# FFT convolution with a mixture-of-experts layer: half of the t stores issued by SP, and the constants loaded by SP

## What is computed

```python
def _attn_ref(x, filt_r, filt_i):          # x: 8 batches x 3072 x 256, float32
    X = np.fft.rfft(x, axis=1)
    Y = X * (filt_r + 1j * filt_i)[None]
    return np.fft.irfft(Y, n=x.shape[1], axis=1)

def _moe_ref(x, w_gate, w1, w2, capacity): # 8 experts, 256 -> 1024 -> 256, capacity 768
    logits = x @ w_gate
    expert_idx = np.argmax(logits, axis=1) # gate_w: softmax weight of that expert
    # each expert takes its first `capacity` rows in order; all other rows stay zero
    h = np.maximum(np.einsum('ecd,edf->ecf', disp, w1), 0.0)
    y = np.einsum('ecf,efd->ecd', h, w2)
    # out[i] = gate_w[i] * y[expert, slot] for rows that were kept
```

## Time and profile before

| | |
|---|---|
| three runs | 547.15, 548.21, 555.39 us |
| profiled execution | 550.09 us |
| its span, first to last instruction | 548.3 us |
| mean granted TensorE clock | 0.963 of full |
| busy: TensorE, its weight loads | 472.4 (86%), 376.8 us (69%) |
| busy: VectorE, ScalarE, GpSimd | 222.1 (41%), 205.8 (38%), 216.8 us (40%) |
| moved by DMA | 119.72 MB, mean 218 GB/s |

### The profile page before, as it was taken

One profiled execution on the slowest core, in us unless ns is written; L12 is line 12 of the kernel. 1 busy time (PEld: TensorE's weight loads), 2 busy tenths in 40 slices (PEclk: granted clock), 3 DMA queues, 4 the chain that ended last, 5 costly groups with the idle time before them and its releaser, 6 DMA issues.

```text
span 548.3 us, 9488 instructions
## 1 busy us (share of the span) xinstructions
PE 472.4 (86%) x3806; PEld 376.8 (69%) x3806; DVE 222.1 (41%) x335; ACT 205.8 (38%) x362; POOL 216.8 (40%) x190
## 2 busy tenths in 40 slices
PE   5446666999988986989888998999999999999994
PEld 1123223245544553459888998999999999998994
DVE  7025103233344579757925522253413434232210
ACT  2301322345533633445215444253633535243221
POOL 7080100000000000274545778755678565775212
PEclk9959979899998999999999999999999999999998
DMA  8989978889759646799931316943069331491001
GB/s 285 334 311 408 409 255 264 286 291 298 254 185 340 217 153 210 237 391 405 364 111 40 123 41 238 390 135 133 30 233 394 132 116 49 158 362 58 30 22 43
DMA packets 64532, 119.72 MB, mean 218 GB/s; under 512 B 7760, under 2 KB 35296, under 8 KB 64480
## 3 DMA queue, kind: packets, MB, share of 16 engines
q1 hardware_dynamic: 33168, 70.95, 36.8%
q0 software_dynamic: 9824, 25.33, 12.8%
q10 hardware_dynamic: 21488, 22.75, 12.2%
HBM read 60.78 MB, written 58.23 MB: 217 GB/s over the span
## 4 chain that ended last, share of the span: by engine, by line
PE 62%; DMA 13%; DVE 8%; issue 6%; ACT 5%; ACTq 3%; SPq 2%; POOL 0%; POOLq 0%; DVEq 0%
PE back L1288 21%; PE wide L1274 10%; PE bank L1274 10%; PE back L484 6%; PE low L517 4%; DMA t_scratch<-t_out 4%; DMA u_scratch<-v_out 3%; PE low L499 3%; PE wide L471 3%; ACTq L681 2%; DVE pq L796 2%; PE low L652 2%; PE bank L532 2%; ACT t_out L674 2%; DMA w_raw<-in_w 1%
## 5 line engine op out<-in xcount | busy, mean ns | idle before, releaser
L1288 PE MATMUL back<-w2h,hh 128*128 128x256 f32 x384 | 109.7, 286 | 0.0
L1288 PE MATMUL back<-w2l,hh 128*128 128x256 f32 x384 | 108.6, 283 | 0.0
L1288 PE MATMUL back<-w2h,hl 128*128 128x256 f32 x384 | 108.6, 283 | 0.0
L796 DVE TENSOR_TENSOR pq<-wide,fab 128x1024 f32<-128x1024 f32 x45 | 55.0, 1223 | 123.8 <-PE wide L471 119.1
L1099 DVE SCALAR_TENSOR_TENSOR hl<-wide,hh 128x384 fp32r<-128x384 f32 x64 | 34.7, 555 | 119.6 <-ACT hh L1051 83.6
L1188 POOL DMA_INDIRECT out<-o_out,token x48 | 50.5, 1052 | 81.5 <-ACT o_out L1060 60.4
L1288 PEld LDWEIGHTS back<-w2l,hh 128*128 128x128 f32 x384 | 73.6, 192 | 0.1
L1288 PEld LDWEIGHTS back<-w2h,hl 128*128 128x128 f32 x384 | 73.6, 192 | 0.0
L1288 PEld LDWEIGHTS back<-w2h,hh 128*128 128x128 f32 x384 | 73.6, 192 | 0.0
L1160 POOL DMA_INDIRECT g_in<-y_rows,token x48 | 52.6, 1095 | 33.1 <-DVE token L967 17.4
L1060 ACT ACTIVATE o_out<-back,o_gate 128x256 f32<-128x256 f32 x48 | 22.9, 476 | 102.1 <-PE back L1288 97.4
(11 more groups left out here) (131 smaller groups left out, 778.8 us busy)
## 6 DMA issues: line engine op xcount, KB each, us to landing
out<-zero SPq DMA_DIRECT2D x24, 1024.0 KB
w_raw<-in_w SPq DMA_DIRECT2D x14, 1024.0 KB
u_scratch<-v_out ACTq DMA_DIRECT2D x48, 192.0 KB, 4.0
t_scratch<-t_out ACTq DMA_DIRECT2D x30, 256.0 KB, 6.9
z_in<-t_scratch SPq DMA_DIRECT2D x24, 256.0 KB, 3.9
x_in<-in_x POOLq DMA_DIRECT2D x12, 512.0 KB, 15.1
x_in<-in_x SPq DMA_DIRECT2D x6, 512.0 KB, 6.2
z_in<-t_scratch SPq DMA_DIRECT2D x24, 128.0 KB, 4.9
```

What stands on the lines that cost most here:

```text
L796: nc.vector.tensor_tensor(pq[:, n % 3], spectrum(t, h)[:, :, 0, :].unsqueeze(2).to_broadcast([P, 2, 2, D]), fab[:, h], ALU.mult).then_inc( ...
L1288: mm = nc.tensor.matmul(ps[4 + (b * ST + s) % 2][:, 0:D], hx[:, b % 2, f, s * P:(s + 1) * P], wt[:, k, f, :], start=(f == 0 and m == 0), s ...
```

## The change

The second of the two t stores of every chunk (a = 1, the odd partitions) is issued by SP and no longer by ScalarE, and the five loads of constants as well. SP waits for the same count of t_evac as ScalarE does. Batch 0's six stores stand on SP behind table group 0; those of batch 1 lie around z_load(0, 7), those of batch 2 in steps g = 0 to 2 of stage 1, with the v loads behind the third. The constants are issued after the last store of batch 1 and ahead of z_load(1, 0).

```diff
+        def t_store(eng, t, c, a):
+            at = a * 32 + c * 2 * CH if c < 4 else A1 + a * 16 + (c - 4) * 2 * CH
+            buf = v_in if t == 0 and c >= 3 else t_out
+            eng.wait_ge(t_evac, t * 12 + 2 * c + 2)
+            dst = zt[t, at:at + 2 * CH].rearrange("(n r) (p d) -> (r p) n d", r=2, d=D)
+            eng.dma_start(dst, buf[a:P:2, c % 3]).then_inc(t_written[c % 3], 16)
+
+        def t_stores(sp, t, first, last):
+            for c in range(first, last):
+                t_store(sp, t, c, 1)
...
+        def load_constants(sp):
+            sp.wait_ge(set_up, SET_UP)
+            sp.nop(nofuse=True)
+            sp.dma_start(wai[:, :], wai_d).then_inc(consts, 16)
+            sp.dma_start(sq[:, :, :], sq_d).then_inc(consts, 16)
+            sp.dma_start(wgs[:, :, 0:E], wg.rearrange("(h p) e -> p h e", p=P)).then_inc(consts, 16)
+            sp.dma_start(rows[:, :, :], row_d).then_inc(consts, 16)
+            sp.dma_start(nums[:, :], num_d).then_inc(consts, 16)
+
         def sp_stage(sp, t, ai):
+            late = A_FROM[t] > 0
             for g in range(NG):
                 n = g + ZB
+                if not late:
+                    if g == 0:
+                        t_stores(sp, t + 1, 0, 1)
+                    elif g == 1:
+                        t_stores(sp, t + 1, 3, 4)
+                    elif g == 2:
+                        t_stores(sp, t + 1, 4, NCH)
+                elif n == NG - 1:
+                    t_stores(sp, t + 1, 0, 2)
+                elif n == NG:
+                    t_stores(sp, t + 1, 2, NCH)
+                if t == 0 and n == NG:
+                    load_constants(sp)
                 if n < NG:
                     z_load(sp, t, n)
                 else:
                     z_load(sp, t + 1, n - NG)
+                if not late and g == 0:
+                    t_stores(sp, t + 1, 1, 3)
                 if ai is not None:
...
             if h == 1:
-                act.wait_ge(t_evac, t * 12 + i + 1)
-                for a in range(2):
-                    at = a * 32 + c * 2 * CH if c < 4 else A1 + a * 16 + (c - 4) * 2 * CH
-                    dst = zt[t, at:at + 2 * CH].rearrange("(n r) (p d) -> (r p) n d", r=2, d=D)
-                    act.dma_start(dst, buf[a:P:2, c % 3]).then_inc(t_written[c % 3], 16)
+                t_store(act, t, c, 0)
...
                 load_tables(sp, 0)
+                t_stores(sp, first, 0, NCH)
                 sp.wait_ge(gaps_set, r + 1)
...
-                def stage(t, a, ai, rt):
-                    act_stage(act, t, a, ai, rt)
-                    if t == 0:
-                        act.dma_start(sq[:, :, :], sq_d).then_inc(consts, 16)
-                        act.dma_start(wai[:, :], wai_d).then_inc(consts, 16)
-                        act.dma_start(wgs[:, :, 0:E], wg.rearrange("(h p) e -> p h e", p=P)).then_inc(consts, 16)
-                        act.dma_start(rows[:, :, :], row_d).then_inc(consts, 16)
-                        act.dma_start(nums[:, :], num_d).then_inc(consts, 16)
-                stages(first, last, stage)
+                stages(first, last, lambda t, a, ai, rt: act_stage(act, t, a, ai, rt))
```

## The result

Over twenty runs of each kernel, the changed one has a median of 546.58 us and the kernel before 550.85 us. The ratio is 0.9918, with a 95% interval of 0.9892 to 0.9944: a gain of 4.5 us, where 6.6 were forecast. The ratios leave out executions more than 1.5% above the shortest of the same kernel, the medians count all. Three more sets of runs, on three chips, gave 0.9973 [0.9934, 1.0011], 0.9959 [0.9923, 0.9995] and 0.9921 [0.9884, 0.9959]. The mean of the four is 0.9943, some 3.1 us. Two sets of the kernel before against itself gave 1.0032 and 0.9973, so a single set doesn't tell 0.3% from nothing. The changed kernel is faster, by a little under half of what was forecast.

What follows compares the result with a forecast made beforehand. Transfers and their issue were taken to set the pace before 117 us, TensorE's own work behind it. 0.9 + 4.0 + 1.7 = 6.6 us off the median of 548.21 gave 541.6 us, range 535 to 547.5.

Steps and rivals of the forecast that it cites:

- Batch 0: 0 to 27 us: fewer store issues on ScalarE bring the last landing earlier; 0.9 us, ends 0 and 2.9.
- the slack of 1.1 us: End of batch 0: the DMA work left at 24 us could be done by 25.8, 1.1 us ahead of the landing.
- Stage 0: Batch 1, 57 to 91 us: halves in two queues release chunk 3's copy 5.0 us earlier; gain 4.0 us, ends 1.0 and 6.9.
- SP's issue of the constants: After batch 1's last store: ends by 82 us, five microseconds ahead of the landing, and costs nothing; without that cover, 4.1 us.
- Stage 1: Batch 2, 95 to 117 us: one store issue less per chunk removes most of TensorE's waits; 1.7 us, ends 0 and 3.5.
- rival B: Both clock dips, in stage 0 and at the start of stage 1, shrink too: 12.6 us gained, 535.6 us; chance 0.16.
- the move of the constants: Start of stage 1: taking the constants off ScalarE looks like 4 us and is nothing, as TensorE works without a gap.
- the sum: Whole kernel: 0.9 + 4.0 + 1.7 = 6.6 us gained, all before 117 us.
- Behind 117 us: From 117 us to the end: the path is TensorE's own work, so the earlier gain comes out nearly whole.
- A: Stage 0: landings stay, since all transfers share 16 DMA engines; only shorter issues gain, 1.0 us there; 544.6 us; chance 0.25.
- C: Stage 1: a longer wait keeps the clock at 1.2 GHz through batch 2; 4.9 us slower, 553 us; chance 0.06.
- The bound of 2%: Whole kernel: a difference under 2% (11 us) is about what can't be told from no change; chance of that 0.82.

Runs made afterwards that it cites:

- consts_back: The changed kernel with the five loads of constants back on ScalarE at the end of stage 0; 0.9898 of the kernel before, median 555.54 us.
- busy_last: The changed kernel with three unused TensorE products of 512 columns added in the last stage; 0.9896 of the kernel before, median 542.73 us.
- all_on_sp: The changed kernel with both t stores of every chunk issued by SP, none by ScalarE; 0.9963 and 0.9871 of the kernel before in two sets.

## Why the prediction went as it did

**Batch 0, forecast 0.9 us, measured 0.1.** The first z load is at 27.25, 27.26, 26.97 and 26.98 us, before at 27.12, 27.23 and 27.19. ScalarE's part came nearly as worked out (last issue at 20.66 instead of 22.97, 2.3 us where 2.9 were worked out), the engines were full, and the last stores took 6.4 us instead of 4.0. What failed in this term is the slack of 1.1 us that I saw between the work left at 24 us and the landing: with the stores issued earlier, the share from 24 to 27 us is still 0.58 (0.61 before), and the landing stays. That one slow engine among the 16 is waited for would explain it, but is not shown.

**Stage 0, forecast 4.0 us.** The rows fit the mechanism, the halves in two queues and ScalarE's ending last; but batch 0 alone, with both halves in one queue, has part of the gain, so it isn't shown to be the whole cause. The sizes were off. SP's half took 8.3 us, not 6, and ScalarE's 10.0 and more, not 8.4. Chunk 3's release is at 68.03, 69.79, 68.73 and 68.84 us, 3.3 us earlier in the mean than 72.44, 72.65 and 71.44, where 5.0 were forecast. The z load is 3.6 us earlier in the mean (6.0 in the first profile, 1.9 to 3.6 in the others, against the mean of before, 91.4), where 4.9 were forecast, batch 0 included. SP's issue of the constants, forecast to end by 82 us, ended at 87.4 and 88.3 in the third and second profiles, 1.2 to 1.3 us ahead of the z load: it still cost nothing, but with no 5 us to spare.

**Stage 1, forecast 1.7 us, measured 3.5.** From z load to wai the four profiles take 21.02, 22.14, 21.97 and 24.08 us, mean 22.3; before 25.8. My sum kept the dip at 96 to 100 us. It was absent in three of four, so rival B's term was real here; and with it gone, the move of the constants, costed at nothing, began to count, as `consts_back` has it. The part alone (25.33 us) is worth nothing, as forecast: the error was to cost it for the schedule before and not for the one that the rest of the change makes.

**Up to 117 us** this adds up to 7.1 us in the mean and 5.8 without the first profile, close to the 6.6 of the sum, by terms that err in both directions: the sum was near by luck. `busy_last` is the same kernel up to there and has both old dips (0.50 in 72 to 76 and in 96 to 100 us) and 114.50 us; with it the mean is 6.2 us.

**Behind 117 us, forecast 0.** Here the prediction failed: "what is won before 117 us should therefore come out of the end nearly whole". In the last three profiles 2.3 us are gone by the first w_raw load, in last stages of 114.2 to 116.8 us instead of 113.6. What is left there, 3.5 us, agrees with the 3.1 us of the timed sets; with the lucky first profile it would be 5.6. The step that failed is the reading of the path: TensorE's being busy for 30 of 30 us in stage 1 said nothing of the last stage, where it waits for v and for VectorE. The chain of the kernel before shows that wait, in two transfers that the earlier trace rows stops short of:

```profile
157.82 2.89 DMA u_scratch<-v_out
161.32 4.92 DMA x_in<-u_scratch
```

Behind it the granted clock fell to 0.74 from 164 to 168 us already then. So the term of the last stage was put at nothing without a look at it; it came out at 1.4 us against the change in the mean of four profiles. Why the clock falls deeper or twice in some executions of the changed kernel stays open.

**The rivals.** A had the size nearest to the median, for a wrong reason: its landings were to stay, and chunk 0's pair released the copy at 68.0 to 69.8 us instead of 71.4 to 72.6. B's two dips are gone in three of four profiles, but a low window stands at 76 to 84 us in their place (0.57 in the first, 0.50 in the second and third), and only the first execution (540.95 us) comes near B's side. C wasn't seen in stage 1. The bound of 2% for what can be told was also too coarse: four sets of runs tell 0.6% from nothing, and a faster kernel was to be expected with that forecast.

**Open:** what batch 0's order does to stage 0, and with it how much of the earlier landing is due to the second queue; why the wait for v in the last stage is 0.3 us longer in three of four profiles, and what lets the clock fall there; and the 1.0077 of batch 1 alone.

## What to carry to other kernels

When a store's landing is on the path, look at what stands ahead of it in its own queue, and try the later half in a queue that is empty at that moment: with the DMA engines full, the pair then landed 9.3 to 11.7 us after its first issue instead of 13.2 to 15.6. How much of that is the queue's and how much the order of earlier stores, these runs don't separate. Cost each part of a change in the schedule that the other parts make; a cover made of slow work goes when the work gets fast. Read the chain of waits to its end before a later stretch is put at nothing. And when executions of one kernel differ by more than the change, read several profiles, note how far each lies from its median, and compare milestones, not one span.

## What was not expected of the hardware

The kernel's spread (540.95 to 554.08 us in twenty runs) is that of TensorE's granted clock (0.970 to 0.950). An idle time of 2.8 us in front of the last stage's products was followed by no low window in one execution, and one of 3.1 us by windows of 0.50 to 0.67 in two others; but 3.08 us with only the constants moved by none, and 2.50 us in `all_on_sp` by 0.77. Thirteen unused products kept the clock up only while they ran; it fell in the next 4 us, at a busy time of 1.72 us.
